# Where the small loads, the first maxima and the last pair's quotients are done in a linear-attention and two-MoE kernel

## What is computed

```python
def phi(x):
    proj = einsum('bhsd,df->bhsf', x, w_phi)
    proj = proj - max(abs(proj), axis=-1, keepdims=True)
    return concatenate([exp(proj), exp(-proj)], axis=-1)
q_p, k_p = phi(q), phi(k)                      # (4, 8, 576, 256)
kv = einsum('bhsf,bhsd->bhfd', k_p, v)
z = sum(k_p, axis=2)
x = einsum('bhsf,bhfd->bhsd', q_p, kv) / (einsum('bhsf,bhf->bhs', q_p, z)[..., None] + 1e-06)
x = x.transpose(0, 2, 1, 3).reshape(2304, 512)
# first MoE, dense: every one of 8 experts sees every row
P = exp(x @ w_gate - max);  8 rounds of row and column normalisation
out = sum over e of P[:, e:e+1] * (maximum(x @ w1[e], 0) @ w2[e])
# second MoE, routed: cosine scores over tau, argmax, one expert for each row
out[mask] = gate_w[mask, None] * (maximum(x[mask] @ w1[e], 0) @ w2[e])
```

## Time and profile before

| | us |
|---|---|
| median of 3 runs | 2082.79 (2082.35 to 2082.95) |
| profiled execution | 2086.45 |
| its span, first to last instruction | 2084.7 |
| TensorE busy | 2040.1 (98%) |
| VectorE busy | 1018.4 (49%) |
| ScalarE busy | 686.7 (33%) |
| GpSimd busy | 179.7 (9%) |
| mean granted TensorE clock | 0.992 |

### The profile page before, as it was taken

The page is one execution under the profiler, slowest core; times in us unless marked ns, Lnnn a source line. Parts: engine busy times, 40 slices in busy tenths (PEclk is TensorE's granted clock), DMA queues, the critical chain, the costliest instruction groups (busy, mean ns, idle before and its releaser), DMA issues.

```text
span 2084.7 us, 31677 instructions
## 1 busy us (share of the span) xinstructions
PE 2040.1 (98%) x12658; PEld 1210.5 (58%) x12658; DVE 1018.4 (49%) x1610; ACT 686.7 (33%) x1354; POOL 179.7 (9%) x183
## 2 busy tenths in 40 slices
PE   6999899999999999999999999999999999899998
PEld 5788655555555555555555555555555565567775
DVE  6888755544444444444444444444444432644343
ACT  3566443322322333322322333322323322222221
POOL 0553400000000000000000000000000000211110
PEclk9999999999999999999999999999999999999999
DMA  6233111122122112212211221122122240641600
GB/s 200 64 69 69 47 41 41 41 106 97 41 81 81 41 41 81 88 63 93 82 41 41 81 81 41 68 96 80 41 81 81 82 182 21 253 162 45 259 36 8
DMA packets 93103, 169.38 MB, mean 81 GB/s; under 512 B 60438, under 2 KB 60566, under 8 KB 89760
## 3 DMA queue, kind: packets, MB, share of 16 engines
q1 hardware_dynamic: 88960, 157.92, 21.5%
q0 software_dynamic: 4000, 9.45, 1.4%
HBM read 126.19 MB, written 44.83 MB: 82 GB/s over the span
## 4 chain that ended last, share of the span: by engine, by line
PE 96%; DVE 2%; issue 1%; DMA 0%; ACT 0%; POOL 0%; SPq 0%; POOLq 0%; DVEq 0%
PE ps L639 36%; PE ps L658 36%; PE ps L839 6%; PE ps L823 4%; PE ps L588 3%; PE ps L601 3%; PE ps L825 2%; PE ps L567 2%; PE ps L576 1%; PE ps L554 1%; PE ps L703 1%; PE ps L794 1%; DMA tau_sb<-in_moe_tau_dram 0%; PE ps L673 0%; DVE vmp L1155 0%
## 5 line engine op out<-in xcount | busy, mean ns | idle before, releaser
L639 PE MATMUL ps<-arena 128*128 128x384 f16 x4608 | 778.2, 327 | 3.6 <-ACT arena L939 3.4
L658 PE MATMUL ps<-arena 128*128 128x512 f16 x3456 | 772.2, 380 | 0.0
L639 PEld LDWEIGHTS ps<-arena 128*128 128x128 f16 x4608 | 451.5, 98 | 317.6 <-issue 4.0
L658 PEld LDWEIGHTS ps<-arena 128*128 128x128 f16 x3456 | 339.0, 98 | 393.0 <-issue 3.6
L935 ACT ACTIVATE arena<-ps 128x384 f32<-128x384 f32 x384 | 188.5, 491 | 1031.7 <-PE ps L639 1019.0
L1215 DVE TENSOR_TENSOR arena<-arena 128x384 f16<-128x384 f32 x384 | 214.2, 558 | 319.2 <-ACT arena L939 318.1
L1270 DVE SCALAR_TENSOR_TENSOR arena<-ps,wt,arena 128x512 f32<-128x512 f32 x126 | 94.6, 751 | 437.4 <-PE ps L658 437.0
L939 ACT ACTIVATE arena<-ps 128x384 f16<-128x384 f32 x384 | 185.9, 484 | 0.0
L1106 DVE TENSOR_REDUCE wg<-arena 128x1 f32<-128x1024 f32 x128 | 154.9, 1212 | 29.0 <-DMA arena<-in_moe_w_dram 28.9
L1122 DVE SCALAR_TENSOR_TENSOR arena<-arena,wsc 128x1024 f16<-128x1024 f32 x124 | 158.4, 1278 | 1.7 <-ACT arena L909 1.6
L909 ACT ACTIVATE arena<-arena,wsc 128x1024 f16<-128x1024 f32 x124 | 142.5, 1150 | 1.9 <-DVE wsc L1053 1.9
(11 more groups left out here) (199 smaller groups left out, 1190.9 us busy)
## 6 DMA issues: line engine op xcount, KB each, us to landing
arena<-in_moe_w_dram SPq DMA_DIRECT2D x32, 2048.0 KB, 9.6
split_weights<-arena SPq DMA_DIRECT2D x16, 2048.0 KB, 7.4
arena<-split_weights SPq DMA_DIRECT2D x8, 4096.0 KB, 13.7
arena<-in_q_dram SPq DMA_DIRECT2D x16, 288.0 KB, 3.5
arena<-in_k_dram SPq DMA_DIRECT2D x16, 288.0 KB, 3.9
arena<-in_v_dram SPq DMA_DIRECT2D x1, 4608.0 KB, 15.0
x_rows<-arena SPq DMA_DIRECT2D x18, 256.0 KB, 2.4
arena<-in_v_dram SPq DMA_DIRECT2D x32, 128.0 KB, 2.3
```

What stands on the lines that cost most here:

```text
L639: last = pe.matmul(o, ring[:, slot, sw, FF * c + 128 * j:FF * c + 128 * j + 128], xT[:, sx, c, BLK * blk:BLK * blk + BLK], start=(n == 0), ...
L658: last = pe.matmul(ps[:, Y_PS + tt, :], hbuf[:, blk % 2, sh, f, 128 * tt:128 * tt + 128], ring[:, slot, 2 + sw, D * f:D * f + D], start=(n ...
```

## The change

It has two parts that touch no common instruction.

The first is in the opening: SP issues the values of pairs 0 and 1 ahead of the three small loads. VectorE takes the gate maximum, with its wait for these loads, in pair 1's group 0 instead of pair 0's group 0. The four maxima of the first weights, one in each of the first four groups before, stand as two behind pair 0's group 2 and one each behind pair 1's groups 0 and 1.

The second is at the end of attention: GpSimd leaves the last pair out. VectorE multiplies its quotient and scale in one instruction for columns 0 to 384 and one for 384 to 576 between the reciprocals, ScalarE copies each to its fp16 high part, and VectorE subtracts for the low parts; then comes `gate_scale`. ScalarE and TensorE wait for 15 of `xsplit_done` and for the new `last_split`.

```diff
+        RECIP = (0, 4 * S // 6, 5 * S // 6, S)
+        LAST = ((0, RECIP[1]), (RECIP[1], S))
+        X_LAST = xT[:, :, H // 2 - 1, N - S:N]
...
             load_raw(0, w1a_v[0])
+            sp.wait_ge(vone_done, 5)
+            load_v(0, 0)
+            load_v(1, 1)
             sp.dma_start(gate_raw[:, :, :], w_gate.rearrange("(c p) e -> p c e", p=128)).then_inc(small_in, 16)
             sp.dma_start(emb_sb[:, :], emb).then_inc(small_in, 16)
             sp.dma_start(tau_sb[:, :], tau.partition_broadcast(128)).then_inc(small_in, 16)
-            sp.wait_ge(vone_done, 5)
-            load_v(0, 0)
-            load_v(1, 1)
             sp.dma_start(vall, vall_v).then_inc(vall_in, 16)
...
+                    if i == PAIRS - 1:
+                        break
...
-                    pe.wait_ge(xsplit_done, PAIRS)
+                    pe.wait_ge(xsplit_done, PAIRS - 1)
+                    pe.wait_ge(last_split, 1)
                     pe.wait_ge(gate_cut, 1)
...
-            act.wait_ge(xsplit_done, PAIRS)
+            for n, (n0, n1) in enumerate(LAST):
+                act.wait_ge(last_scaled, n + 1)
+                act.activation(X_LAST[:, 0, n0:n1], num[:, 1, n0:n1], ACT.Copy).then_inc(last_hi, 1)
+            act.wait_ge(xsplit_done, PAIRS - 1)
+            act.wait_ge(last_split, 1)
...
-                        if first and par == 0 and g == 0:
+                        if first and par == 1 and g == 0:
                             dve.wait_ge(small_in, 16 * 3)
...
-                        if first and par == 0:
-                            largest(0, g)
+                        if first and par == 0 and g == 2:
+                            largest(0, 0)
+                            largest(0, 1)
                         if first and par == 1:
-                            if g == 0:
-                                largest(0, WP - 1)
+                            if g < 2:
+                                largest(0, 2 + g)
                             values_max(2 * g, 2 * g + 2)
...
-            for g in range(GP):
-                invert(PAIRS - 1, g, 1)
+
+            def last_quotients(n):
+                n0, n1 = LAST[n]
+                dve.wait_ge(recip_done, GP * (PAIRS - 1) + (1, GP)[n])
+                dve.wait_ge(num_ready, 2 * PAIRS)
+                dve.scalar_tensor_tensor(out=num[:, 1, n0:n1], in0=num[:, 1, n0:n1], scalar=xsc[:, 0:1],
+                                         in1=den[:, 1, n0:n1], op0=ALU.mult, op1=ALU.mult).then_inc(last_scaled, 1)
+
+            invert(PAIRS - 1, 0, 1)
+            last_quotients(0)
+            invert(PAIRS - 1, 1, 1)
+            invert(PAIRS - 1, 2, 1)
+            last_quotients(1)
+            for n, (n0, n1) in enumerate(LAST):
+                dve.wait_ge(last_scaled, n + 1)
+                dve.wait_ge(last_hi, n + 1)
+                ins = dve.tensor_tensor(X_LAST[:, 1, n0:n1], num[:, 1, n0:n1], X_LAST[:, 0, n0:n1], ALU.subtract)
+            ins.then_inc(last_split, 1)
             gate_scale()
```

More of the change, by code:

```diff
@@ L228, in moe_attention_kernel @@
         xsplit_done = sem("xsplit_done")
+        last_scaled, last_hi, last_split = sem("last_scaled"), sem("last_hi"), sem("last_split")
         vpart_done = sem("vpart_done")
@@ L288, in moe_attention_kernel @@
         SPLIT = {1: 0, 2: 1, 3: 2, 4: 3}
-        RECIP = (0, 4 * S // 6, 5 * S // 6, S)
         SPAN = SLOTS // 4
```

## The result

| | before | changed |
|---|---|---|
| median of 16 runs, us | 2083.13 (2079.77 to 2085.33) | 2077.88 (2075.67 to 2079.32) |
| profiled execution, us | 2086.45 | 2078.09 |
| its span, us | 2084.7 | 2076.3 |
| mean granted TensorE clock | 0.992 | 0.994 |

The ratio is 0.9973, 95% interval 0.9966 to 0.9979: the change makes the kernel 5.3 us faster by the medians (4.4 to 7.1 by the interval), 8.4 us by the two profiled executions. The forecast was 2074.3 with a range of 2070.5 to 2079.0, so the time lies inside, but 3.6 us over the point, outside the forecast's own range of 2072 to 2077.5, and nearer to what rivals 1 and 2 give (2076.7 and 2078.1).

The account below looks back on a forecast made before the run. TensorE bounds 96% of the span, with gains where it waits: the opening's VectorE chain (1.3 us) and the MoE's start (7.2). Their 8.5 us off 2082.79 gave 2074.3, range 2070.5 to 2079.

Parts of the forecast that it names:

- rival 1: Opening: gives nothing or loses, as the big load lands 1.55 us later; -1.1 there, 2076.7 in all; chance 0.12.
- rival 2: MoE's start: the clock falls all the same, keeping 3.9 us of slow matmuls; 2078.1; chance 0.10.
- The last quotients: End of attention: ScalarE starts the hidden rows at 253.85 instead of 257.33, and TensorE's idle 3.38 us are gone.
- what is late next: MoE's start: the last of VectorE's four L1122 ends at 272.6, setting the first output; the MoE start gains 7.2 us.
- The clock term of the sum: MoE's start: with no idle time the clock doesn't fall, saving 2.03 + 1.83 us of slow matmuls.
- The opening's landing: Opening: the big load's landing shifts by -0.3 us (bounds -0.7 and +1.55) to 31.6, a gain of 2.1.
- The stretch behind: Opening, after the first values' maxima: gives back 0.74 us for the fourth weight maximum and 0.06 for the low clock.
- One of the signs for wrong: Opening: a first L1155, the values' maxima, later than 33 would show the forecast wrong.
- rival 3: Routing stage: its clock comes out differently; 2071.6 if the fall goes, 2077.0 if a second group meets one; chance 0.12.
- rival 4: Opening: slower, the low clock from near 34 us lasting into the stretch from 60; 2089 if held for 30; chance 0.03.
- rival 5: End of attention: VectorE's new chain ends where GpSimd's did (257.3); MoE part 0, time 2081.5; chance 0.03.

Follow-up runs that it names:

- the filler: Kernel before with 14 unread matmuls of 512 columns in TensorE's idle time at the MoE's start: 2081.28 us against 2084.26, ratio 0.9989.
- opening-alone: Kernel before with only the opening's edit, the last pair on GpSimd as it was: 2082.76 us against 2084.26, ratio 0.9996.
- the filler at 54: Changed kernel with 12 unread matmuls in TensorE's 3.2 us of idle time ahead of the projection at 57.34: 2076.86 us, ratio 0.9972 against the kernel before.

## Why the prediction was right, and where it was off

**The last quotients and what is late next: right.** Forecast 7.2 us from the same point to the first output, 7.26 in the traces. All eleven profiles of kernels with the moved quotients have 24.51 or 24.52 us there, so rival 2 came in none. ScalarE started the hidden rows 5.88 us after the first reciprocal's start (254.88 - 249.00), where I had 5.81 (253.85 - 248.04). The new product took 0.62 and 0.42 where I had 0.56 and 0.35. `gate_scale` took 1.3 us (254.71 to 256.00) where I had 1.2, and VectorE's last L1133 ended 0.25 us ahead of TensorE, where the sum had it 0.03 behind (272.6 and 272.57). On GpSimd's part in it: the 128x1 product took 1.14 us in all three profiles with GpSimd busy beside it, and ended within 0.02 us of GpSimd's L469; with GpSimd still it took 0.16. The Trainium skill's rule of the exclusive port pair ("SBUF — State Buffer", section "SBUF: two separate sides"), which locks the pair for the whole instruction, fits that row. It doesn't fit the next one: L1172 started 0.25 us behind GpSimd's L473 (253.48 + 1.73) and ended at 254.27, 0.94 us ahead of it, slowed (0.54 against 0.25) but not locked out.

**The clock term of the sum: mis-sized.** The step by which the clock falls in the idle time, and twelve matmuls take 4.02 us and twelve 3.82 against 1.99, was right in mechanism, as the filler shows. Its size, 3.86 us, was that of one execution in which the clock stayed low for 10 us. The filler puts it at 2.3 us over the runs, and the opening-alone trace shows an execution with 1.39. The filler's interval, 0.4 to 4.2, still takes in 3.86, so that it was too large on the whole rests on the second trace and on the medians too. By 2.3 it is 1.6 of the missing 3.2 us (8.5 forecast, 5.3 measured); the opening below is 1.0, and 0.6 is within the noise. I made the sum against the profiled execution, which lay 3.66 us over the three runs' median, and didn't ask whether that distance was part of the term.

**The opening's landing: wrong.** The shift of the landing, taken at -0.3 because the 3.54 us were the larger row, failed. The load landed at 32.66 (17.24 + 15.42), 0.79 later than before, and at 33.58 (18.28 + 15.3) in the opening-alone kernel. The 1.5 us of the three issues were right. The 2 us set against them were 1.2, and I overlooked that before the change these issues lay where SP had to wait for VectorE anyway. (My early end was not worked out either: 2 less 1.55 is 0.45 and not 0.7.) The stretch behind came out at 0.78 (24.65 against 23.87) where I had 0.80, but not by its parts: with the fourth maximum taken out, 0.19 of it went and not 0.74, since TensorE's low clock, which I had put at 0.06, held up nearly as much. That the two sums agree is luck.

So the opening had 1.04 - 0.78 = 0.26 us in this profile, instead of 1.3. Over the four profiles with the old opening the projection came at 56.65 to 57.74, over the four with this one (the filler at 54 among them) at 57.16 to 58.37: on the whole no gain at all. The repeated changed kernel says what bound it. There VectorE was ready for the load 2.9 us sooner than in the first profile and waited 7.01 us instead of 3.80:

```profile
33.03 2.61 DVE L1167 TENSOR_REDUCE vmp<-arena 128x1 f32<-128x1152 f32 x2 [7.01 <-DMA arena<-in_v_dram]
```

Its projection came at 57.67 all the same. The new wait was named and the place right, and rival 1, that the opening gives nothing, held, with half of its 1.55 us of later landing. One of the signs for wrong, first maxima later than 33, came in two profiles (33.03 and 33.66).

**What neither part caused.** The changed kernel's profile lost 1.2 us to a low clock near 58 (191.66 us from that projection to the first reciprocal, 190.44 before). It came out 1.65 us better between the first output and the start of the group behind the routing stage's slow one (1487.73 against 1489.38): its L664 took 6.88 where L658 took 7.86 in the earlier trace rows, and L709 had 0.67 less:

```profile
1753.70 6.88 PE ps L664 x24
```

The 0.26 and 7.26 gained, the 1.2 lost and this 1.65 make 8.0 of the 8.4; the other 0.4 lies behind 1761 and was not followed up. Of eight profiles with the idle 3.2 us near 54 left empty, five have a low clock behind it, three of them with the old opening. Of all fourteen, six have a low clock in the routing stage (that group takes 6.46 to 7.86 us there and 5.20 in the other eight), before and changed among them. That is rival 3 in a wider form: it is at several joints, and it goes both ways from profile to profile. The Trainium skill ("TensorE: Matmul & The Clock Gate", section "What's actually happening") calls the gate's window free-running. The traces fit that, with 3.4 us or 10 us of low clock behind one idle gap of the same code, but none shows where the window lay, so this cause is argued and not shown. Rivals 2, 4 and 5 didn't come about.

## What to carry to other kernels

A wait that is taken away in front of a long load is worth only the time up to that load's landing: look up the landing before counting the wait, and look whether the issues that you move lay in a stretch where the issuing engine stood anyway. Then give the load more time, which was worth 4 us here where the edit itself was worth nothing, and see what is queued behind the load. A short chain on two engines can replace a longer one on a slow engine at the end of a stage, and there the gain is the idle time of TensorE plus what its clock loses by it. Size the second part over several executions: of two profiles here one held 1.4 us and the other 3.8, around some 2.3 over the runs.

## What was not expected of the hardware

After one and the same idle gap of 3.4 us TensorE's granted clock was low for 10 us in one execution and for 3.4 in another, which cost 3.83 and 1.39 us. Fourteen matmuls that nothing reads, in the gap, kept it full. Executions of one kernel spread over 3.7 to 5.6 us in 16 runs each. And with the three small loads taken from the front of SP's queue, its block of three to four microseconds moved to another issue: the value issues took 7.8 to 9.2 us over ten profiles, where they took 8.7 to 9.4 over four. Why the queue blocks for that long was not settled; no run here took the first weights' load out of it.
